# Score products over two passes, their operands moved by DMAs: a fused attention and two-mixer kernel on one core

## The reference

```python
# attention: B=2 batches, H=8 heads, S=768, D=64; 4 sink keys, window of 128
scores = scale * np.matmul(q, k.transpose(0, 1, 3, 2))
keep = is_sink | in_window                 # first 4 keys, or 0 <= query - key < 128
scores = np.where(keep, scores, -1e9)
scores = scores - scores.max(-1, keepdims=True)
a = np.exp(scores)
a = a / (a.sum(-1, keepdims=True) + 1e-9)
x = np.matmul(a, v)                        # laid out as (B, S, 512)
# mixer 1 (rank 32 token mixing, 2048 hidden channels), then mixer 2 (256 token, 1536 channels)
h = xt @ U @ V;             u = x + h.T;  x = u + relu(u @ w_ch1) @ w_ch2
h = relu(xt @ w1) @ w2;     u = x + h.T;  y = u + relu(u @ w_ch1) @ w_ch2
```

## Time and profile before

| | |
|---|---|
| median of 3 runs | 632.86 us |
| the profiled execution | 633.67 us |
| its span | 630.8 us |
| mean granted TensorE clock over the span | 0.997 of full |
| busy: TensorE / VectorE / ScalarE / GpSimd | 616.3 / 352.9 / 325.4 / 402.4 us |
| first batch's attention | from 9 to about 76 us |
| second batch's attention, between mixer 1's products | from about 79 to 224 us |

### The profile page before, as it was taken

How to read it: one execution, slowest core, us unless ns; L and a number is a source line. 1 busy time by engine, 2 the same in 40 slices (tenths; PEclk the granted TensorE clock), 3 DMA queues, 4 the chain that set the end, 5 groups by cost and what they waited for, 6 DMA issues and landing times.

```text
span 630.8 us, 10358 instructions
## 1 busy us (share of the span) xinstructions
PE 616.3 (98%) x3466; PEld 556.6 (88%) x3466; DVE 352.9 (56%) x754; ACT 325.4 (52%) x727; POOL 402.4 (64%) x425
## 2 busy tenths in 40 slices
PE   7899889999999999999999999999999999999997
PEld 6789789999999979999999888899998888999986
DVE  7677664554564545776656732495677227665411
ACT  5667566556545555744544544544453447454321
POOL 8656547978979666565665654567566536666352
PEclk9999899999999999999999999999999999999999
DMA  8463333553343415323223332432324343421152
GB/s 171 101 138 90 90 95 102 134 118 116 88 114 98 151 56 165 100 67 117 85 73 111 103 100 82 131 104 68 117 84 116 106 131 84 150 84 34 51 154 78
DMA packets 88467, 65.59 MB, mean 104 GB/s; under 512 B 43040, under 2 KB 72480, under 8 KB 88416
## 3 DMA queue, kind: packets, MB, share of 16 engines
q1 hardware_dynamic: 88416, 64.95, 36.8%
HBM read 61.52 MB, written 3.15 MB: 103 GB/s over the span
## 4 chain that ended last, share of the span: by engine, by line
PE 87%; DVE 6%; POOL 2%; issue 2%; ACT 2%; DMA 1%; DVEq 0%; ACTq 0%; POOLq 0%
PE bank L1612 33%; PE bank L1366 23%; PE bank L1577 10%; PE bank L1442 4%; PE bank L1412 3%; PE bank L1541 3%; PE bank L1491 3%; PE bank L1422 2%; PE bank L1389 1%; PE bank L1517 1%; DVE masked L1141 1%; PE bank L1472 1%; POOL w_lo L878 1%; PE bank L1604 1%; DVE b_lo L1235 1%
## 5 line engine op out<-in xcount | busy, mean ns | idle before, releaser
L878 POOL TENSOR_TENSOR w_lo<-w_raw,w_hi 128x512 fp32r<-128x512 f32 (+1 forms) x158 | 210.3, 1337 | 138.3 <-ACT w_hi L911 137.3
L911 ACT ACTIVATE w_hi<-w_raw 128x512 fp32r<-128x512 f32 (+1 forms) x158 | 96.6, 618 | 54.1 <-PE bank L1612 35.9
L1612 PE MATMUL bank<-w_hi,hid_hi 128*128 128x512 f32 x216 | 86.4, 400 | 0.0
L1612 PE MATMUL bank<-w_hi,hid_lo 128*128 128x512 f32 x216 | 85.0, 394 | 0.0
L1612 PE MATMUL bank<-w_lo,hid_hi 128*128 128x512 f32 x216 | 84.8, 392 | 0.0
L897 ACT ACTIVATE probs<-masked,neg_max 128x264 f32<-128x264 f32 x96 | 49.5, 516 | 67.4 <-DVE neg_max L1141 66.8
L1612 PE MATMUL bank<-w_hi,y_hid 128*128 128x512 f32 x216 | 71.1, 394 | 0.2
L1141 DVE CUSTOM_DVE_ANT_0 masked<-bank,masks 128x264 f32<-128x264 f32 x96 | 41.1, 429 | 31.7 <-PE bank L1412 28.3
L1442 PE MATMUL bank<-v_nat,probs_T 128*128 128x64 f32 x352 | 50.5, 262 | 1.8 <-DVE probs_T L1156 1.0
L1442 PEld LDWEIGHTS bank<-v_nat,probs_T 128*128 128x128 f32 x352 | 48.5, 192 | 3.4 <-DVE probs_T L1156 1.4
L1612 PEld LDWEIGHTS bank<-w_hi,y_hid 128*128 128x128 f32 x216 | 40.5, 188 | 9.5 <-POOL w_lo L878 1.5
(11 more groups left out here) (177 smaller groups left out, 1501.0 us busy)
## 6 DMA issues: line engine op xcount, KB each, us to landing
w_raw<-in_moe_w_ch_dram SPq DMA_DIRECT2D x144, 256.0 KB, 2.7
w_raw<-in_moe_w_ch_dram SPq DMA_DIRECT2D x20, 512.0 KB, 3.5
q_nat<-in_q_dram SPq DMA_DIRECT2D x12, 256.0 KB, 3.3
k_nat<-in_k_dram SPq DMA_DIRECT2D x12, 256.0 KB, 4.0
v_nat<-in_v_dram SPq DMA_DIRECT2D x12, 256.0 KB, 3.8
out_dram<-o_stage SPq DMA_DIRECT2D x11, 256.0 KB, 3.4
w_raw<-in_moe_w_tok_dram SPq DMA_DIRECT2D x6, 256.0 KB, 2.7
w_raw<-in_moe_w_tok_dram SPq DMA_DIRECT2D x8, 192.0 KB, 2.3
```

What stands on the lines that cost most here:

```text
L878: nc.gpsimd.tensor_tensor(w_lo[:, split % NW, 0:n], w_raw[:, split % NR, 0:n], w_hi[:, split % NW, 0:n].bitcast(f32), ALU.subtract) \
L911: nc.scalar.activation(w_hi[:, split % NW, 0:n], w_raw[:, split % NR, 0:n], ACT.Copy) \
L1612: last = mm(m_tile(use)[:, :], stationary, w[:, slot, :], start=False, stop=(final and n == 2), skip_group_check=True)
```

## The change

From tile 2 on (TWO_PASSES_FROM) the scores are made of two products in place of three; before, this was so from tile 6 on. The rows that the two VectorE casts (q_both) and the two ScalarE copies (k_hi) filled are now filled by DMAs from SBUF to SBUF that SP issues at qsplit and ksplit, two per operand and tile, and six small ones once for the sink columns. The products of one head alone (all three of tiles 0 and 1; high by low from tile 2 on) run over the 64 rows of that head in place of 128 rows with zeros, so that only the block "before" tile 0 has still to be zeroed. GpSimd's q_lo is two subtractions of 64 rows from tile 2 on.

```diff
+    TWO_PASSES_FROM = 2
 ...
         def queries_split(T):
-            return T + 1 if T < NQ else 2 * (T + 1) - NQ
+            return T + 1 if T < TWO_PASSES_FROM else 2 * (T + 1) - TWO_PASSES_FROM
         def query_low(eng, wait, T):
-            if T >= NQ:
+            if T >= TWO_PASSES_FROM:
                 for e in range(2):
 ...
+            def move_queries(T):
+                sp.wait_ge(q_high, T + 1)
+                for e in range(2):
+                    rows, there = slice(e * D, (e + 1) * D), slice((1 - e) * D, (2 - e) * D)
+                    sp.dma_start(q_both[there, T % 2, :, e, :].bitcast(f32), q_hi[rows, T % 2, :, :].bitcast(f32)) \
+                      .then_inc(q_there[T % 2], 16)
+            def move_keys(T):
+                sp.wait_ge(k_high, T)
+                for e in range(2):
+                    rows, there = slice(e * D, (e + 1) * D), slice((1 - e) * D, (2 - e) * D)
+                    sp.dma_start(k_hi[there, :, e, T % 3, 0:P].bitcast(f32), k_hi[rows, :, e, T % 3, 0:P].bitcast(f32)) \
+                      .then_inc(k_there[T % 2], 16)
+            def move_first_sinks():
+                sp.wait_ge(k_first_high, 2)
 ...
+                elif s[0] == "qsplit" and s[1] >= TWO_PASSES_FROM:
+                    move_queries(s[1])
+                elif s[0] == "ksplit" and s[1] >= TWO_PASSES_FROM - 1:
+                    if s[1] == TWO_PASSES_FROM - 1:
+                        move_first_sinks()
+                    move_keys(s[1])
 ...
-            for part in (slice(0, 3, 2), slice(1, 2)):
-                nc.gpsimd.memset(k_lo[:, :, :, part, :].rearrange("p a b s k -> p (a b) s k").bitcast(f32), 0.0) \
-                  .then_inc(klo_zeroed, 1)
 ...
+            nc.gpsimd.memset(k_lo[:, :, :, 2, 0:P].rearrange("p a b k -> p (a b) k").bitcast(f32), 0.0) \
+              .then_inc(klo_zeroed, 1)
 ...
-                elif s[0] == "ksplit" and s[1] >= NQ:
-                    T = s[1]
-                    act.wait_ge(k_copied, T + 1)
-                    act.wait_ge(scores_ready, H * (T - 1))
-                    for e in range(2):
-                        src = list(key_parts(k_hi, T))[e][0]
-                        last = nc.scalar.activation(k_hi[(1 - e) * D:(2 - e) * D, :, e, T % 3, 0:P], src, ACT.Copy)
-                    last.then_inc(k_moved, 1)
 ...
-                    if T >= NQ:
-                        for e in range(2):
-                            rows, there = slice(e * D, (e + 1) * D), slice((1 - e) * D, (2 - e) * D)
-                            moved = nc.vector.tensor_copy(q_both[there, T % 2, :, e, :], q_full[rows])
-                        moved.then_inc(q_moved, 1)
 ...
-                        if T >= NQ:
-                            pe.wait_ge(q_moved, T - NQ + 1)
-                            pe.wait_ge(k_moved, T - NQ + 2)
+                        if T == 0:
+                            pe.wait_ge(khi_zeroed, 1)
+                            pe.wait_ge(klo_zeroed, 1)
+                        if T == TWO_PASSES_FROM:
+                            pe.wait_ge(k_there[(T - 1) % 2], 32)
+                            pe.wait_ge(ksinks_there, 96)
+                        if T >= TWO_PASSES_FROM:
+                            pe.wait_ge(q_there[T % 2], 32 * (T // 2))
+                            pe.wait_ge(k_there[T % 2], 32 * ((T + T % 2) // 2))
+                        if T == NQ:
+                            pe.wait_ge(k_moved, 1)
 ...
+                    every, own = slice(0, P), slice(h % 2 * D, (h % 2 + 1) * D)
                     high, low = q_hi[:, T % 2, h // 2, :], q_lo[:, T % 2, h // 2, :]
-                    if T < NQ:
-                        passes = ((high, k_hi), (high, k_lo), (low, k_hi))
+                    if T < TWO_PASSES_FROM:
+                        passes = ((high, k_hi, own), (high, k_lo, own), (low, k_hi, own))
                     else:
-                        passes = ((q_both[:, T % 2, h // 2, h % 2, :], k_hi), (high, k_lo))
-                    for n, (queries, ks) in enumerate(passes):
-                        last = mm(bank[:, 0:NK], queries, keys(ks, T, h // 2, h % 2),
+                        passes = ((q_both[:, T % 2, h // 2, h % 2, :], k_hi, every), (high, k_lo, own))
+                    for n, (queries, ks, rows) in enumerate(passes):
+                        last = mm(bank[:, 0:NK], queries[rows], keys(ks, T, h // 2, h % 2)[rows],
                                   start=(n == 0), stop=(n == len(passes) - 1))
```

More of the change, by code:

```diff
@@ L423, in attention_then_two_mixers @@
         klo_zeroed = sem("klo_zeroed")
+        q_there = [sem(f"q_there{i}") for i in range(2)]
+        k_there = [sem(f"k_there{i}") for i in range(2)]
+        ksinks_there = sem("ksinks_there")
         x2_added = sem("x2_added")
@@ L439, in attention_then_two_mixers @@
         q_high = sem("q_high")
-        q_moved = sem("q_moved")
         k_moved = sem("k_moved")
@@ L697, in load_chunk @@
                 sp.dma_start(dst, src).then_inc(w_loaded[c % NR], 16)
+            def move_queries(T):
[12 more added lines that the diff above has]
+                sp.wait_ge(k_first_high, 2)
+                for e in range(2):
+                    rows, there = slice(e * D, (e + 1) * D), slice((1 - e) * D, (2 - e) * D)
+                    for ring in range(3):
+                        sp.dma_start(k_hi[there, :, e, ring, P:BLK].bitcast(f32),
+                                     k_hi[rows, :, e, ring, P:BLK].bitcast(f32)) \
+                          .then_inc(ksinks_there, 16)
             load_qk(0)
@@ L769, in _ @@
                                     base=0, pattern=[[-1, P]], channel_multiplier=1).then_inc(ident_ready, 1)
-            for part in (slice(0, 3, 2), slice(1, 2)):
-                nc.gpsimd.memset(k_lo[:, :, :, part, :].rearrange("p a b s k -> p (a b) s k").bitcast(f32), 0.0) \
-                  .then_inc(klo_zeroed, 1)
-                if part.start == 0:
-                    nc.gpsimd.memset(masks[:, :, :], 0.0).then_inc(masks_built, 1)
-                    nc.gpsimd.memset(sink_raw[0:HS], 0.0).then_inc(vsink_zeroed, 1)
+            nc.gpsimd.memset(masks[:, :, :], 0.0).then_inc(masks_built, 1)
+            nc.gpsimd.memset(sink_raw[0:HS], 0.0).then_inc(vsink_zeroed, 1)
+            nc.gpsimd.memset(k_lo[:, :, :, 2, 0:P].rearrange("p a b k -> p (a b) k").bitcast(f32), 0.0) \
+              .then_inc(klo_zeroed, 1)
             built = 1
@@ L916, in _ @@
                     act.wait_ge(q_split, queries_split(T - 1))
-                    if T > NQ:
-                        act.wait_ge(q_moved, T - NQ)
                     act.wait_ge(tp_ready, tp_at[s] + 1)
@@ L925, in _ @@
                         act.wait_ge(k_split, keys_split(T - 1))
-                    if T > NQ:
-                        act.wait_ge(k_moved, T - NQ + 1)
                     act.wait_ge(tp_ready, tp_at[s] + 1)
@@ L931, in _ @@
                 elif s == ("ksplit", 0):
-                    act.wait_ge(khi_zeroed, 2)
                     act.wait_ge(k_copied, 1)
@@ L1060, in _ @@
         def _(dve):
-            for part in (slice(0, 3, 2), slice(1, 2)):
-                nc.vector.memset(k_hi[:, :, :, part, :].rearrange("p a b s k -> p (a b) s k").bitcast(f32), 0.0) \
-                  .then_inc(khi_zeroed, 1)
+            nc.vector.memset(k_hi[:, :, :, 2, 0:P].rearrange("p a b k -> p (a b) k").bitcast(f32), 0.0) \
+              .then_inc(khi_zeroed, 1)
             def low_of(key, rows, dst, hi, relu=False):
@@ L1099, in _ @@
                     nc.vector.tensor_copy(q_hi[:, T % 2, :, :], q_full).then_inc(q_high, 1)
-                    if T >= NQ:
-                        for e in range(2):
-                            rows, there = slice(e * D, (e + 1) * D), slice((1 - e) * D, (2 - e) * D)
-                            moved = nc.vector.tensor_copy(q_both[there, T % 2, :, e, :], q_full[rows])
-                        moved.then_inc(q_moved, 1)
                 elif s == ("ksplit", 0):
-                    dve.wait_ge(klo_zeroed, 2)
                     for e in range(2):
@@ L1113, in _ @@
                     dve.wait_ge(k_copied, T + 1)
-                    if T == 1:
-                        dve.wait_ge(khi_zeroed, 2)
                     if T >= 2:
```

## The result

The changed kernel takes 667.86 us (median of 663.07, 663.12, 672.6 and 672.7) where the kernel before took 632.97 beside it (632.5 to 633.94): ratio 1.0551, interval 1.0471 to 1.0631. The forecast was 634.9, range 629.2 to 638.5; what happened is rival 2, which had a chance of 0.06.

A forecast was written before the change was run, and what follows sets the result against it. TensorE bounds the kernel (98% busy), with the chain through GpSimd's q_lo, VectorE's casts and x_nat at tile ends; +3.4 - 1.8 - 0.4 + 0.8 = +2.0 us on 632.86 gives 634.9 us, range 629.2 to 638.5.

The forecast's parts named there:

- rival 2: TensorE drains between product heights: at least 0.17 us a change, two per unit, 80 units, 27 us, 660 us; chance 0.06.
- Does a 64-row product cost more?: Score products on TensorE: taken as 0 extra, from a 96-row product starting 0.12 us after a 128-row one.
- tiles 0 and 1 keep three products, now of 64 rows: First batch's tiles 0 and 1: as many columns, so the same 0.12 us per product.
- The clock: TensorE idles before tile 5's "down", so the clock falls before work it limits: +0.8 us, between 0 and 1.5.
- The held casts: Ends of tiles 1 to 4: VectorE's k_hi casts wait for GpSimd's two q_lo subtractions, delaying x_nat: +3.4 us, bounds 0 to 4.2.
- The product removed: Tiles 2 to 5, 32 units at 0.12 us, 3.84 in all; 1.80 counts where TensorE is the limit: -1.8 us.
- tile 5: q_both casts gone, but k_hi casts still wait for the q_lo pair: -0.4 us, bounds 0 and -3.0.
- No difference in the second batch but the shift: Sign of being right: from 90 to 210 us the changed kernel differs only by the shift.
- Rival 1: Tiles 1 to 4: casts slip in between the two q_lo subtractions, the 3.4 us vanish, 630.7 us; chance 0.27.
- Rival 3: Keys arrive late by DMA (1.27 us issue, 2.5 landing); 1 us more costs 4 tiles 0.6 each, 637.3 us; chance 0.06.

The follow-up runs named there:

- the bursts: Kernel before with bursts of 264-column products of various row heights appended after its last output; 760.65 us in total, pairs 128/64 0.32 us start to start.
- e4: Changed kernel with every product over 128 rows, two products from tile 2 (tile 2 has an extra third), sink columns moved per ring slot: 635.02 us, ratio 1.0037.
- e10: e4 with the high by low product over the head's own 64 rows from tile 2 on: 654.8 us, ratio 1.0352.
- e8: Kernel before with GpSimd's q_lo subtraction of tiles 2 to 5 split into two of 64 rows: 636.27 us, ratio 1.0048.
- e3: Kernel before with only the second batch's q_both and k_hi halves (tile 6 on) filled by SP's DMAs: 634.26 us, ratio 1.0012.
- e5: e4 with GpSimd's second q_lo subtraction put behind the first half of k_lo: 632.67 us, ratio 0.9994.
- e9: e5 with the sink-column moves issued ahead of the queries: 632.95 us, ratio 0.9994.
- e1: Kernel before with only its single-head products run over that head's 64 rows: 685.18 us profiled, the other three runs 706.8 to 707.2.
- e7: Kernel before with dense bursts appended, height changing only between bursts (128, 64, 96 rows, pairs of lower and upper 64): pairs 0.12 us, total not given.

## Why the prediction was wrong, point by point

- **The step that failed: "Does a 64-row product cost more? ... I take 0."** It costs nothing among its like (0.12 us) and 0.39 us a unit where it stands alone between 128-row ones; so "tiles 0 and 1 keep three products, now of 64 rows ... the same 0.12 us" failed with it. The row I leaned on was a real measurement of the wrong thing: 96 rows cost no change, 64 and 32 do (the bursts). I had argued from "fewer than 128" when the row only showed "96". The Trainium skill's page TensorEngine Tiling (Array Packing), section Key Properties, had the rule that a change of tiling mode drains TensorE, and its section Tiling Modes lists row tiles of 128, 64 and 32, and none of 96. By that list my row could not speak against the rule. The runs agree with rule and list: 0.20 us a change for 64 and 32 rows, none seen for 96.
- **Rival 2** had the mechanism and nearly the sum: 27 us and 660, from 0.17 a change. Measured 0.19 to 0.20 of delay at each change; that it is a drain of TensorE is the page's word, the traces show the delay. It is 30.6 us in the profiled execution because tiles 0 and 1, which it left out, cost 8.1 more, and what `e4` loses without any 64 rows is 1.8 (632.6 against 630.8), while the 80 units from tile 2 on cost 20.4 (of 80 x 0.39 = 31; in the first batch they use up idle time before "down": only 4.0 of the 20.4 us are there by the end of tile 5, 75.47 in `e10` against 71.45 in `e4`). So that 27 and 28.8 lie so near is in part luck: it had the 80 units too dear and tiles 0 and 1 at nothing. What was wrong above all was its chance.
- **The clock.** I watched for falls in idle stretches. The largest one came where the profile calls TensorE 100% busy.
- **The rest of the sum came out near, in part by luck.** `e4` is the change without its 64 rows: 635.02 (+1.9 against 633.13 beside it), where the sum said 634.9 (+2.0). The held casts, +3.4: 3.1 measured alone. The product removed, tile 5 and the clock, -1.8 - 0.4 + 0.8 = -1.4: from `e8` to `e4`, 636.27 to 635.02, it is -1.25. But the +0.8 for a fallen clock was not paid there: four of `e4`'s seven runs, the median one and the profiled one among them, have a granted clock of 1.00, while the profiled run of `e8` has such a fall (at 69.5). In its place `e4` holds tile 2's extra product, half as wide as a score product, in 8 units (an estimate from the 0.12 us: some 0.5 us). With the clock at 1.00 my terms give +1.2, and +1.9 was measured. Tile 5 moved x_nat by 0.5 us in `e3` where 0.4 was booked, and nothing of it reached the time. "No difference in the second batch but the shift" held for the DMAs (`e4` is 1.6 us late at "down" in tile 6, 78.95 against 77.32, and 1.8 at the end), but not for the 64 rows.
- **Rival 1** (casts slip in) fell in `e8`. **Rival 3** (late keys) did not occur in the changed kernel, whose units leave the DMAs time; it occurred in tile 3 alone once the casts were no longer held (`e5`, `e9`), and from both sides: in `e9` the issue on SyncE began 2.2 us after the casts' end and took 2.13 us where I had 1.27, and landing took up to 3.3 us where I had 2.5 (in `e5` 3.2 to 4.0).
- **Open:** why the clock falls. Two changes of height around one product did not bring it down (`e10`, profiled run); dense pairs of 128 and 64 did, and so did units with three 64-row products, though these also ran at 1.00 (`e1`, 60 to 70 us). Whether a fall in tiles also needs the heavy DMA traffic there (share 1.03 to 1.20 in tile 0, where the kernel before with 1.03 to 1.16 kept its clock) was not tried; the bursts had none. So within the 8.1 us of tiles 0 and 1 the drain and the clock are not separated by a run. An estimate bounds them: 16 units at 0.39 us (`e1` at full clock) make 6.2 us at most, which leaves some 1.9 or more for the clock.

## What to carry to other kernels

Before products are shortened to the rows that hold data, look at what stands on either side: a 64-row product among 128-row ones costs two changes of 0.2 us and saves nothing: 264 columns took 0.12 us over 64 rows as over 128, so the zeros in the other 64 rows were free. Group products of one height, or leave them all at 128. And a neighbouring row is a bound only for what it shares with the new case: when a rule names classes (128, 64, 32), first ask in which class the row lies. Last, when an engine is at 100% and its count of instructions per us has fallen, read the gaps between starts.

## What the runs showed of the hardware that was not expected

- A change between 128 and 64 rows, or 128 and 32, delays the next product by 0.20 us at full clock (0.32 start to start against 0.12) and by 0.30 at the lower level (0.52 against 0.22); between 128 and 96 by nothing (0.12 in the earlier trace rows, 0.22 in the pairs at the lower level).
- The granted clock fell to 0.50 in stretches that the profile reports as fully busy, in dense pairs of 128 and 64 rows and in tiles whose units hold three 64-row products; it held 1.00 in 15 us of 64-row products without changes (`e7`, 638 to 653).
- Products on rows 0 to 63 and on rows 64 to 127, into two banks, run at the same time: 0.12 us a pair (`e7`).
- GpSimd's tensor-tensor holds VectorE's casts from SBUF to SBUF until it ends, also where the casts start while the second of two runs: 1.71 us for a pair of casts that takes 0.85 alone, ended 0.76 after the subtractions (`e8`; this one was forecast). 64 rows take GpSimd as long as 128, 1.29 us.
